# A three-stage kernel on one core: the feed-forward up-projection by Strassen's seven block products, up and down as separate phases

## The reference

```python
# 1. decayed linear attention: 4 batches x 8 heads, 768 steps, head size 64
state = gamma[None, :, None, None] * state + np.einsum('bhd,bhe->bhde', k[:, :, t], v[:, :, t])
y[:, :, t] = scale * np.einsum('bhd,bhde->bhe', q[:, :, t], state)
# 2. mixture of experts, one of 8 per token: 3072 tokens, 512 -> 1024 -> 512
h = np.maximum(x[mask] @ w1[e], 0.0)
out[mask] = gate_w[mask, None] * (h @ w2[e])
# 3. feed-forward: 512 -> 2048 -> 512
h = x @ w_in
g = h * (1.0 / (1.0 + np.exp(-1.702 * h)))
return (g @ w_out).astype(np.float32)
```

## Time and profile before

| | us |
|---|---|
| median of 3 runs (1022.63 to 1023.19) | 1022.81 |
| profiled execution | 1022.28 |
| its span, first to last instruction | 1020.5 |
| PE busy (97% of the span) | 986.9 |
| PE's share of the chain that ended last | 88% |
| DVE busy | 339.7 |
| ACT busy | 263.5 |
| POOL busy | 273.9 |

### The profile page before, as it was taken

The page is one execution under the profiler, slowest core; times in us unless marked ns, Lnnn a source line. Parts: engine busy times, 40 slices in busy tenths (PEclk is TensorE's granted clock), DMA queues, the critical chain, the costliest instruction groups (busy, mean ns, idle before and its releaser), DMA issues.

```text
span 1020.5 us, 16938 instructions
## 1 busy us (share of the span) xinstructions
PE 986.9 (97%) x6091; PEld 809.4 (79%) x6092; DVE 339.7 (33%) x531; ACT 263.5 (26%) x467; POOL 273.9 (27%) x291
## 2 busy tenths in 40 slices
PE   7999699999999999998999999999999999999995
PEld 5888557888888888887788888888888888888884
DVE  3444374222222222224554332332233233223221
ACT  2333223222222222222122322322232232223221
POOL 4444043710025710004671510140051024001001
PEclk9999989999999999999999999999999999999998
DMA  8778257641236511026730200110020011001001
GB/s 306 237 250 256 77 201 255 226 136 62 73 124 206 165 62 41 22 103 183 253 122 0 84 1 0 42 41 0 0 82 0 0 41 41 0 0 42 1 1 41
DMA packets 37183, 96.38 MB, mean 94 GB/s; under 512 B 5132, under 2 KB 5300, under 8 KB 37124
## 3 DMA queue, kind: packets, MB, share of 16 engines
q1 hardware_dynamic: 16720, 43.02, 13.4%
q0 software_dynamic: 11440, 36.54, 10.7%
q10 hardware_dynamic: 8964, 16.05, 4.5%
HBM read 54.67 MB, written 24.15 MB: 77 GB/s over the span
## 4 chain that ended last, share of the span: by engine, by line
PE 88%; DMA 4%; DVE 3%; issue 2%; POOL 1%; ACT 1%; SPq 0%; ACTq 0%; DVEq 0%; POOLq 0%
PE bank L1242 25%; PE bank L1244 25%; PE bank L1243 25%; PE bank L1147 2%; PE bank L1121 2%; PE bank L1289 2%; PE bank L1137 1%; PE bank L1108 1%; PE bank L1156 1%; DMA raw<-w_in 1%; PE bank L1251 1%; DMA raw<-w_out 1%; PE bank L1324 1%; POOL weights L506 1%; PE bank L1167 1%
## 5 line engine op out<-in xcount | busy, mean ns | idle before, releaser
L1242 PE MATMUL bank<-weights,act_hi 128*128 128x512 f32 x384 | 151.8, 395 | 4.1 <-POOL weights L506 4.0
L1060 DVE TENSOR_TENSOR act_f<-bank,sig 128x512 f32<-128x512 f32 x96 | 66.3, 691 | 260.4 <-ACT sig L776 260.4
L1244 PE MATMUL bank<-weights,act_lo 128*128 128x512 f32 x384 | 150.3, 391 | 0.0
L1243 PE MATMUL bank<-weights,act_hi 128*128 128x512 f32 x384 | 150.1, 391 | 0.0
L1243 PE MATMUL bank<-fT_lo,weights 128*128 128x512 f32 x384 | 149.4, 389 | 0.0
L1242 PE MATMUL bank<-fT_hi,weights 128*128 128x512 f32 x384 | 149.4, 389 | 0.0
L1244 PE MATMUL bank<-fT_hi,weights 128*128 128x512 f32 x384 | 149.4, 389 | 0.0
L776 ACT ACTIVATE sig<-bank 128x512 f32<-128x512 f32 x96 | 57.4, 598 | 295.8 <-PE bank L1244 295.8
L581 POOL DMA_INDIRECT out<-f_out,token_idx x24 | 23.6, 982 | 365.2 <-ACT f_out L647 334.3
L1062 DVE TENSOR_TENSOR act_lo<-act_f,act_hi 128x512 fp32r<-128x512 f32 x96 | 98.3, 1024 | 67.1 <-ACT act_hi L647 67.1
L1242 PEld LDWEIGHTS bank<-weights,act_hi 128*128 128x128 f32 x384 | 72.5, 189 | 19.9 <-POOL weights L506 4.9
(11 more groups left out here) (160 smaller groups left out, 1260.0 us busy)
## 6 DMA issues: line engine op xcount, KB each, us to landing
weights<-raw POOLq DMA_DIRECT2D x32, 512.0 KB, 4.9
qk_in<-qk SPq DMA_DIRECT2D x24, 512.0 KB, 4.6
raw<-w SPq DMA_DIRECT2D x24, 512.0 KB, 5.5
y_slots<-y_out ACTq DMA_DIRECT2D x26, 256.5 KB, 3.7
v_in<-v SPq DMA_DIRECT2D x24, 256.0 KB, 5.2
x_rows<-x_out ACTq DMA_DIRECT2D x24, 256.0 KB, 4.2
raw<-w_in SPq DMA_DIRECT2D x8, 512.0 KB, 6.1
raw<-w_out SPq DMA_DIRECT2D x8, 512.0 KB, 4.0
```

The lines of the kernel that those rows point to most:

```text
L1060: tt(act_f[:, f % 2, :], ps_h[f % 2][:, :], sig[:, f % 2, :], ALU.mult).then_inc(act_done, 1)
L1242: mm(dst, hi, w_hi, start=first, stop=False)
L1243: mm(dst, hi, w_lo, start=False, stop=False)
L1244: return mm(dst, lo, w_hi, start=False, stop=last)
```

## The change

The feed-forward stage works on three groups of 1024 tokens. The up-projection of a group takes `w_in` in eight pieces; piece k holds four blocks of 256 x 128 (two halves of the inner dimension, hidden blocks k and k + 8), and the tokens are two halves of 512. The 2 x 2 x 2 block product is made of seven products (Strassen's scheme in Winograd's form) instead of eight. For that

- POOL forms four combinations of the weight blocks per piece in the first group (`mix`), SP stores the piece of 128 x 2048 to DRAM (`w_comb`), and the two later groups load it from there; ACT and DVE split each piece again in each group (`early_hi`, `late_hi`, `early_lo`, `late_lo`);
- DVE forms four combinations of the token blocks per group (`mix_x`), and ACT and DVE split seven;
- the sums of products are made partly by accumulating in PSUM, partly by ACT copying a bank (`keep_sum`) and DVE adding another (`add_sum`).

A piece ("pair" in the code) has 7 products x 2 blocks x 3 = 42 matmuls of 512 columns. All eight pieces come first, with the activations kept in SBUF (`act_f`); then follows the down phase, two times 16 blocks of 12 matmuls, for which `w_out` comes in pieces of 128 x 1024 through the same three buffers, once per group. The first group fetches 8 token tiles ahead of the stage instead of 4, from `y_head`, which now has 15 tiles. All groups are written out without a loop.

```diff
+            def mix(k):
+                comb = comb_f[k % COMB_BUFS]
+                e = lambda at_: comb[:, at_ * QUAD:(at_ + 1) * QUAD]
+                pool.wait_ge(comb_in[k % COMB_BUFS], DMA_INC * (k // COMB_BUFS + 1))
+                add = nc.gpsimd.tensor_tensor
+                add(e(S1_AT), e(A21_AT), e(A22_AT), ALU.add).then_inc(comb_step, 1)
+                add(e(S3_AT), e(A11_AT), e(A21_AT), ALU.subtract)
+                pool.wait_ge(comb_step, 2 * k + 1)
+                add(e(S2_AT), e(S1_AT), e(A11_AT), ALU.subtract).then_inc(comb_step, 1)
+                pool.wait_ge(comb_step, 2 * k + 2)
+                add(e(S4_AT), e(A12_AT), e(S2_AT), ALU.subtract).then_inc(comb_mixed, 1)
```

The order on POOL around the first group (`fetch` is the gather of rows, of gates, and the scaling, of four token tiles):

```diff
+            mix(0)
+            mix(1)
             hold(y_stored, DMA_INC * used_tiles + DMA_INC * (HEAD_TILES + 1))
+            pool.wait_ge(x_split, PRODUCTS)
+            pool.wait_ge(up_done, 1)
+            fetch(1, range(ROW_BUFS))
+            mix(2)
+            mix(3)
+            mix(4)
+            fetch(1, range(ROW_BUFS, GT))
+            for k in range(5, PAIRS_F):
+                mix(k)
+            store_half(0, 0)
+            store_half(0, 1)
```

SP loads and stores the first group's pieces:

```diff
+            def store_mixed(k):
+                sp.wait_ge(comb_mixed, k + 1)
+                sp.dma_start(w_comb[k], comb_f[k % COMB_BUFS][:, :]).then_inc(comb_stored[k % COMB_BUFS], DMA_INC)
+            load_piece(0, 0)
+            load_piece(0, 1)
+            store_mixed(0)
+            store_mixed(1)
+            for g in range(GROUPS):
+                for k in range(GROUP_PIECES):
+                    if g > 0 or k > 1:
+                        load_piece(g, k)
+                    if g == 0 and 1 < k < PAIRS_F:
+                        store_mixed(k)
```

ACT's order in one piece, and at the start of the down phase:

```diff
+                    if k > 0:
+                        sigmoid_last(g, k - 1)
+                        late_hi(g, k)
+                    keep_sum(g, k, P1, ps_X, 2, done_act + 4 * (k - 1) + 2)
+                    keep_sum(g, k, P5, ps_Y, 1, done_act + 4 * (k - 1) + 3)
+                    keep_sum(g, k, P6, ps_X, 0, done_act + 4 * (k - 1) + 1)
+                    if k + 1 < PAIRS_F:
+                        early_hi(g, k + 1)
+                    else:
+                        out_hi(g, 0)
...
+                    sigmoid_sum(g, k, 0, k, 1)
+                    sigmoid_sum(g, k, 1, k + PAIRS_F, 1)
+                    sigmoid_sum(g, k, 2, k, 0)
+                split_act(g, 0)
+                sigmoid_last(g, PAIRS_F - 1)
```

DVE: the lo of a weight piece's larger part, and the order in one piece:

```diff
+            def early_lo(g, k):
+                piece = GROUP_PIECES * g + k
+                if g == 0:
+                    dve.wait_ge(comb_stored[k % COMB_BUFS], DMA_INC * (k // COMB_BUFS + 1))
+                dve.wait_ge(w_hi_done, early_count(g, k))
+                tt(comb_lo[piece % COMB_BUFS][:, EARLY_AT:], comb_f[piece % COMB_BUFS][:, EARLY_AT:],
+                   w_hi[piece % HI_BUFS][:, LATE:].bitcast(F32), ALU.subtract).then_inc(w_split, 1)
...
+                    if k > 0:
+                        gated(g, k - 1, 2, k - 1 + PAIRS_F, 1, h_sum[:, 1, :])
+                        gated(g, k - 1, 4, k - 1 + PAIRS_F, 0, ps_X[(k - 1) % 2][:, :])
+                        late_lo(g, k)
+                    add_sum(g, k, P3, ps_Y, 0, 3)
+                    add_sum(g, k, P7, ps_X, 1, 2)
+                    if k + 1 < PAIRS_F:
+                        early_lo(g, k + 1)
                     else:
+                        out_lo(g, 0)
+                    add_sum(g, k, P2, ps_Z, 2, 1)
+                    gated(g, k, 1, k, 1, h_sum[:, 0, :])
+                    gated(g, k, 3, k, 0, h_sum[:, 2, :])
```

PE's waits ahead of the seven products of a piece (P1, P5, P6, P3, P7, P2, P4 in this order):

```diff
+                    if product == P1:
+                        pe.wait_ge(w_split, early_count(g, k))
...
+                    if product == P6:
+                        pe.wait_ge(up_copied, 3 * this + 1)
+                    if product == P3:
+                        pe.wait_ge(up_copied, 3 * this + 2)
+                    if product == P7:
+                        pe.wait_ge(up_copied, 3 * this + 3)
+                        pe.wait_ge(w_split, late_count(g, k))
...
+                    if product == P4:
+                        pe.wait_ge(h_ready, 3 * this + 2)
+                    if k == 0:
+                        pe.wait_ge(x_split, PRODUCTS * g + product + 1)
```

More of the change, by code:

```diff
@@ L790, in _, with take_turned @@
-            group(0, True)
-            with act.Fori(1, GROUPS - 1) as n:
-                group(n, True)
-            group(GROUPS - 1, False)
+            def take_turned(g, j):
+                act.wait_ge(fT_done, GT * g + j + 1)
+                side, col = divmod(j, HT)
+                copy(xT4[:, side::2, :, col * P:(col + 1) * P],
+                     ps_fT[j % 2].rearrange("p (a c) t -> p a c t", c=2)).then_inc(fT_copied, 1)
+            for j in range(GT):
+                take_turned(0, j)
+                if j % 2 == 1 and j < GT - 1:
+                    expert_step(READY_TILE + j // 2, False)
@@ new lines, in _, with split_x, early_hi @@
+            for i in range(TILES, 1 + TILE_LOOPS * XG_BUFS):
+                with act.If(used_tiles > i):
+                    expert_step(i, False)
+            def split_x(g, product, src):
+                wait(act, x_mixed, 4 * g + {P1: 0, P5: 1, P6: 2, P3: 2, P7: 3, P2: 3, P4: 4}[product])
+                copy(mix_hi[:, product, :, :], src).then_inc(x_hi_done, 1)
+            def early_hi(g, k):
+                piece = GROUP_PIECES * g + k
+                if g == 0:
+                    act.wait_ge(comb_mixed, k + 1)
+                else:
+                    act.wait_ge(comb_in[piece % COMB_BUFS], DMA_INC * (piece // COMB_BUFS + 1))
+                piece_used(act, piece - HI_BUFS)
+                copy(w_hi[piece % HI_BUFS][:, LATE:], comb_f[piece % COMB_BUFS][:, EARLY_AT:]).then_inc(w_hi_done, 1)
@@ new lines, in sums, with keep_sum, sigmoid, sigmoid_sum @@
+            def sums(g, k, product):
+                return PRODUCTS * (PAIRS_F * g + k) + product + 1
+            def keep_sum(g, k, product, bank, at_, free):
+                act.wait_ge(up_done, sums(g, k, product))
+                wait(act, act_done, free)
+                copy(h_sum[:, at_, :], bank[k % 2][:, :]).then_inc(up_copied, 1)
+            def sigmoid(dst, src):
+                nc.scalar.activation(dst, src, ACT.Sigmoid, scale=1.702).then_inc(sig_done, 1)
+            def sigmoid_sum(g, k, at_, f, side):
+                act.wait_ge(h_ready, 3 * (PAIRS_F * g + k) + at_ + 1)
+                sigmoid(act_f[:, f, side * HALF:(side + 1) * HALF], h_sum[:, at_, :])
```

630 lines of the change are left out of this document (395 added, 235 removed).

## The result

The changed kernel takes 1043.68 us (median of four runs, 1041.5 to 1046.72), the kernel before 1023.0; the ratio is 1.0203, 95% interval 1.0171 to 1.0235: slower beyond the noise, though whether by more than 2% the interval leaves open. The forecast was 1044, range 1026 to 1072. The profiled execution took 1045.54 us with a span of 1043.8, against 1022.28 and 1020.5 before.

A forecast was written before the change was run, and what follows sets the result against it. The prediction took PE, busy 97% of the span, to bound the kernel. A saving of 39.2 us against new waits, port and clock costs summed to +21.1 us, giving 1044 us, with an 8-in-10 range of 1026 to 1072.

The forecast's parts named there:

- products and before's waits: Feed-forward stage: 48 fewer matmuls in each of 3 groups save 32.6 us, the earlier kernel's waits 6.6: 39.2 us at most.
- entry, until P6 of piece 0: Start of the feed-forward stage: PE wants P6 at 475.3, gets it at 481.5 behind ACT's and DVE's splits: 6.2 us.
- wait ahead of piece 2: First group: PE waits 13.6 us for piece 2's weights, behind last tile's store, POOL's fetch, mix, store and lo.
- wait ahead of piece 5: First group: PE waits 9.8 us for piece 5's weights, mixed only after POOL's second fetch of four tiles.
- late adds, table load: After the two long waits DVE and ACT still have adds and sigmoids to do, so P6 comes late: 3 us.
- phase changes: Between up and down: 6.6 us for three changes up to down, 4.6 for two down to up.
- port: Second group: POOL's two scaling bursts of four tiles slow DVE, 2 us each, 4 us together.
- clock: PE runs at a lower clock after eight new waits of 2 us and more: 10 us.
- pieces bound by DVE and ACT: Rival: later hand-overs inside pieces cost 1.2 us more in each of 24 pieces, 1073 us; chance 0.15.
- the store chain at 9.4 us: Rival: with 9.4 us stores the first group's pieces come every 14 us, not 10: 1068 us; chance 0.10.
- no net change: Rival: small waits throughout, no clock loss at phase changes and no port cost, about 1021 us; chance 0.07.
- Weights in time: Rival: POOL's fetch and mixes stay clear of PE, so the two long waits go: 1015 us; chance 0.08.

The follow-up runs named there:

- experiment 7: Changed kernel with POOL's scaling of rows from the third group's fetches on covering one column, not 512 (timing only): 1036.83 us, ratio 1.0147 to the kernel before.
- experiment 3: Changed kernel with the first two activation blocks split inside piece 7, ahead of its last adds: 1033.72 us, ratio 1.0119 to the kernel before.
- experiment 1: Changed kernel with all eight w_in pieces loaded, mixed and stored during the expert stage: 1017.7 us, ratio 0.9952 to the kernel before.
- 2: Changed kernel with only mix(2) moved ahead of POOL's wait for the last tile's rows and the fetch: 1036.87 us, ratio 1.0134 to the kernel before.
- 8: Changed kernel with each row scaled behind the next row's gate fetch, not in one burst, in the third group's fetches: 1040.2 us, ratio 1.0181.
- Experiment 5: Changed kernel with SP issuing the store of piece 0 ahead of the load of piece 1: 1041.06 us, ratio 1.0171 to the kernel before.
- experiment 4: Changed kernel with conditional expert steps nested on PE, ACT and DVE, so unused ones take one jump, not five: 1043.13 us, ratio 1.0216.

## Why the prediction was right

The mechanism held: the long waits, their chain and the way of the result came as forecast. That the sum came within 1 us is in part luck: the entry was put 5.8 us too low and the phase changes 5.6 too high, and the two errors cancel. By the prediction's own terms; the measured end of the last product is 1031.7 us, 22.7 later than before.

| term | forecast | measured | how |
|---|---|---|---|
| products and before's waits | -39.2 | -39.2 | products by the last group's up phase, 76.7 us; before's waits as read |
| P6 inside pieces | +2.5 | +1.3 | 0.4 us in a group without other waits, x3 |
| entry, until P6 of piece 0 | +6.2 | +12.0 | P6 at 487.3, not 481.5; due at 475.3 |
| wait ahead of piece 2 | +13.6 | +12.9 | rows above |
| wait ahead of piece 5 | +9.8 | +10.7 | rows above |
| late adds, table load | +3 | +1.5 | pieces 2 to 4 and 5 to 7, less their slow clock |
| phase changes | +11.2 | +5.6 | three of 1.85; none from down to up |
| port | +4 | +4.0 to 4.7 | experiment 7 |
| clock | +10 | +11.1 | six stretches of 1.7 to 2.4 from P6 of piece 0 on; one more, of 1.4, lies inside the entry |
| sum | +21.1 | +19.9 to 20.6 | |

The remaining 2 to 3 us are mostly the down phases: 88.0 us each even without a wait behind it (experiment 3), where 384 x 0.2267 gives 87.05. Of the signs of being right that the prediction named, two did not show: the wait ahead of P6 in piece 0 was 2.05 us and not 6, since PE itself came late, and PE did not wait from down to up.

- **The two long waits**: right in cause, by experiments 1 and 2, and within 1 us in size in this trace; in 3, 7 and 8, equal up to there, the two are 14.9 to 15.0 and 9.4 to 11.8. The sizes are partly luck. The chain's start was 5.6 us later than forecast (tile stored at 486.3, not 480.7), but PE reached piece 2 later too, so the difference stayed. Link by link: the tile's store 4.5 us (3.7), the fetch 18.7 (18.1), mix 2.9 (3.2), store 4.8 (5.5), lo and hand-over 1.3. Two figures of the working don't follow from the rows and intervals it names: piece 5 due at 544.2 (512.5 + 10.4 + 10.4 + 9.5 is 542.8), and the store's bounds of 4.2 and 9.4 us.
- **The entry**: the step failed, in its start and not in its kind. I had DVE begin its row at 468.9 with ACT's first hi, and had said that the first two pieces cost nothing, because their loads could go in time. I left out their stores: SP issues the store of piece 0 only behind the load of piece 1, so it went at 466.5 and DVE waited until 475.4. Experiment 5 shows it, and 2 us of its cost. ACT, too, began late, at 469.95 and not 467.8:

```profile
469.95 1.06 ACT L745 ACTIVATE w_hi<-comb 128x1024 fp32r<-128x1024 f32 x1 [2.35 <-issue]
```

DVE could have begun behind that hi, at 471.0: 2.1 of its 6.5 us of delay come from ACT and 4.4 from the store, and its row was 0.7 shorter than the 10.7 forecast. The other thing missed was PE's 8.5 us in jumps over the code of unused tiles (with 1.4 of slow clock behind them it began piece 0 at 482.4 and not 472.6), which cost nothing measurable in this version by experiment 4, because both delays lay side by side.
- **Phase changes**: up to down 1.85 us against 2.2 forecast. Down to up was a misreading: the next piece's buffer is free two blocks before the end, not one; ACT's two hi copies started at 681.7, 5.3 us ahead of the first product of up at 686.99, and PE went on without a gap. So 4.6 us were charged too many. The rows of ACT and PE:

```profile
681.70 1.79 ACT L745 ACTIVATE w_hi<-comb 128x1024 fp32r<-128x1024 f32 x2 [2.15 <-PE bank L1507]
```

```profile
686.99 0.40 PE L1505 MATMUL bank<-mix_hi,w_hi 128*128 128x512 f32 x1
```

- **Port**: 2 + 2 us forecast, 2.38 + 1.61 measured, and shown by 7 and 8. The Trainium skill, "SBUF — State Buffer", section "Who interferes with whom", has such operations of DVE and POOL exclude each other for an instruction; the 5.28 us for three products beside a burst, against 2.07 without, agrees. That both bursts could count in full did not come about, since pieces had slack for the rest.
- **Clock**: 10 forecast, 11.1 measured by distances between products of 0.43 instead of 0.2267 us. The two rows are from the changed kernel, behind the wait of 1.86 us at 773.91:

```profile
775.45 0.63 PE L1505 MATMUL bank<-w_hi,act_hi 128*128 128x512 f32 x1
775.88 0.63 PE L1506 MATMUL bank<-comb_lo,act_hi 128*128 128x512 f32 x1
```

- **The store of 1 MB**: landed after 4.8 us in the chain ahead of piece 2 and after 4.8 to 5.1 in seven of the eight stores; only that of piece 0, issued 0.4 us behind the load of piece 1, took 8.9. I took 5.5. By the page that the prediction cited, the Trainium skill, "DMA: Bandwidth & Descriptors", section "Bandwidth", 8.2 us had been the estimate; the measurement decides.
- **Rivals**: pieces bound by DVE and ACT is refuted by 76.7 us for eight pieces; the store chain at 9.4 us by 4.8 us; no net change by the interval of the ratio. "Weights in time" was worked out at 1015 us; the kernel that makes it true, experiment 1, took 1017.7.

## What to carry to other kernels

A change that takes arithmetic off the bounding engine is worth only what its new inputs let through: here 32.6 us of products were saved and 55 us net of waits and slow clock came in (22.7 + 32.6), 26 of them from one decision, to prepare weights behind a fetch on the same in-order engine while that engine had time in the stage before. Walk every queue that a prepared block passes, stores too, and ask at each entry what its wait is queued behind. And before a stall is removed, look for the one that lies beside it: removing five jumps gave back nothing, since the next wait ended at the same moment.

## What was unexpected of the hardware

- PE idled 8.5 us, with nothing to wait for in the profile, ahead of the last tile, behind five untaken blocks of some 60 products each, 1.7 us a block; nested into one jump it was 2.9 us, and 1.2 more a little later. The Trainium skill, "Runtime: NRT & Kernel Launch", section "Instruction fetch mechanics", says that a taken branch to code that isn't loaded yet waits for its fetch; the rows fit that, though no run here separates the fetch from other costs of a branch. POOL idled 15.6 us in its loop over unused tiles ahead of mix(0).
- A wait of 1.85 us at the same place was followed by nine products at the lower clock in some executions and by none in others: behind all three changes from up to down in the changed kernel, behind only one of three in experiment 1. The slow clock is thus a term with a chance, not a fixed price per wait.
